# Attention, experts and FFN on one core: block sums one slot later, the first weights' load and its parts moved, ScalarE's order in step 1 changed

## The reference

```python
k_sum = k.reshape(B, H, nb, 32, D).max(axis=3)      # nb = 24 blocks of 32 keys
v_sum = v.reshape(B, H, nb, 32, D).mean(axis=3)
# scores: 1/8 q k^T where |i-j| < 16, else -1e9; and 1/8 q k_sum^T + log(32)
# softmax over both, times [v, v_sum]            -> x (1536 tokens, 512)
out = sum_e p[:, e] * (relu(x @ w1[e]) @ w2[e])     # 4 experts, hidden 1024
h = out @ w_in ; g = h * sigmoid(1.702 h) ; result = g @ w_out   # hidden 2048
```

## Time and profile before

| | |
|---|---|
| median of three runs | 845.85 us |
| the profiled execution's own time | 845.02 us |
| its span | 843.2 us |
| TensorE busy | 818.9 us |
| attention of the first sequence (slots) | 0 to 50.5 us |
| steps 0 and 1 on TensorE | 50.5 to 86.9 us |
| steps 2 to 47 and the end | 86.9 to 843.2 us |

### The profile page before, as it was taken

The page is one execution under the profiler, slowest core; times in us unless marked ns, Lnnn a source line. Parts: engine busy times, 40 slices in busy tenths (PEclk is TensorE's granted clock), DMA queues, the critical chain, the costliest instruction groups (busy, mean ns, idle before and its releaser), DMA issues.

```text
span 843.2 us, 13851 instructions
## 1 busy us (share of the span) xinstructions
PE 818.9 (97%) x5014; PEld 805.1 (95%) x5014; DVE 542.0 (64%) x1194; ACT 399.1 (47%) x859; POOL 555.5 (66%) x414
## 2 busy tenths in 40 slices
PE   5896999999999999999999999999999999999998
PEld 4786999999999999999999999999999999999998
DVE  6896666656665566566566666666676665665665
ACT  3863544544444454434334344444455555454541
POOL 3685566656566699756656578877578887466450
PEclk9978999999999999999999999999999999999999
DMA  9981216142112112212213112112112112322102
GB/s 265 277 218 57 92 54 216 51 149 73 51 63 108 51 51 93 77 51 98 72 51 108 62 51 101 51 50 101 51 51 101 50 55 96 126 68 84 51 1 76
DMA packets 26420, 74.72 MB, mean 89 GB/s; under 512 B 14704, under 2 KB 15856, under 8 KB 20208
## 3 DMA queue, kind: packets, MB, share of 16 engines
q1 hardware_dynamic: 26352, 73.84, 26.9%
HBM read 70.66 MB, written 3.17 MB: 88 GB/s over the span
## 4 chain that ended last, share of the span: by engine, by line
PE 89%; POOL 3%; SPq 3%; issue 1%; DMA 1%; DVE 1%; ACT 1%; DVEq 0%; ACTq 0%; POOLq 0%
PE bank L1146 29%; PE bank L1148 29%; PE bank L1147 29%; DMA v_cols<-v_t 1%; PE bank L1101 1%; SPq L404 1%; PE bank L1138 1%; PE bank L1112 1%; SPq L411 1%; POOL wd_lo L543 0%; POOL wd_lo L559 0%; POOL xb_other_lo L567 0%; POOL w_sum L520 0%; SPq L422 0%; SPq L417 0%
## 5 line engine op out<-in xcount | busy, mean ns | idle before, releaser
L948 DVE TENSOR_TENSOR xa<-bank,xa 128x384 f32<-128x384 f32 x352 | 195.8, 557 | 220.0 <-PE bank L1148 215.6
L1146 PE MATMUL bank<-h_hi,wd_hi 128*128 128x384 f32 x768 | 257.8, 336 | 0.1
L1148 PE MATMUL bank<-h_lo,wd_hi 128*128 128x384 f32 x768 | 257.4, 335 | 0.0
L1147 PE MATMUL bank<-h_hi,wd_lo 128*128 128x384 f32 x768 | 257.3, 335 | 0.0
L543 POOL TENSOR_TENSOR wd_lo<-stage,wd_hi 128x1024 fp32r<-128x1024 f32 x47 | 112.5, 2393 | 169.1 <-ACT wd_hi L714 169.1
L755 ACT ACTIVATE h_hi<-bank 128x384 fp32r<-128x384 f32 x192 | 94.3, 491 | 226.0 <-DVE bank L981 178.7
L1146 PEld LDWEIGHTS bank<-h_hi,wd_hi 128*128 128x128 f32 x768 | 144.7, 188 | 1.2 <-issue 1.2
L1147 PEld LDWEIGHTS bank<-h_hi,wd_lo 128*128 128x128 f32 x768 | 144.7, 188 | 0.0
L1148 PEld LDWEIGHTS bank<-h_lo,wd_hi 128*128 128x128 f32 x768 | 144.7, 188 | 0.0
L531 POOL TENSOR_TENSOR wu_lo<-stage,wu_hi 128x1024 fp32r<-128x1024 f32 x47 | 112.6, 2396 | 0.0
L1146 PE MATMUL bank<-xb_other_hi,wu_hi 128*128 128x384 f32 x336 | 112.3, 334 | 0.3 <-ACT snap L739 0.3
(11 more groups left out here) (79 smaller groups left out, 1283.2 us busy)
## 6 DMA issues: line engine op xcount, KB each, us to landing
stage<-weights SPq DMA_DIRECT2D x48, 1024.0 KB, 4.9
k_win<-k_w SPq DMA_DIRECT2D x8, 720.0 KB, 8.9
v_win<-v_w SPq DMA_DIRECT2D x8, 576.0 KB, 9.1
q_bd<-q_t SPq DMA_DIRECT2D x16, 192.0 KB, 8.8
p_bc<-p_rows SPq DMA_DIRECT2D x8, 384.0 KB, 4.8
v_cols<-v_t SPq DMA_DIRECT2D x6, 384.0 KB, 6.0
out<-xa SPq DMA_DIRECT2D x4, 384.0 KB, 7.5
out<-xa SPq DMA_DIRECT2D x8, 192.0 KB, 1.9
```

Of the source, the lines that this page charges most:

```text
L948: nc.vector.tensor_tensor(at, y_bank(g, t), at, ALU.add).then_inc(y_taken, 1)
L1146: nc.tensor.matmul(dst, w_h, a_h, start=first, stop=False, skip_group_check=True)
L1147: nc.tensor.matmul(dst, w_l, a_h, start=False, stop=False, skip_group_check=True)
L1148: return nc.tensor.matmul(dst, w_h, a_l, start=False, stop=last, skip_group_check=True)
```

## The change

Four edits; the instructions stay the same, their order changes.

1. **Block sums of values.** A new list `values_due(slot, lag)` sets the slots: the sum of unit u > 0 goes from slot 3u+1 to 3u+2, the turn and the mean from 3u+2 to 3u+3; the spread stays in 3u+4. Unit 0 is unchanged.
2. **Weights of pair 0.** Their load is issued behind `v_cols` and `v_win` of unit 3 and no longer ahead of them. `high_raw(0)` goes from slot 10 to slot 12, `low_first(0)` and `(1)` from slots 11, 12 to 13, 14, `high_down(0, *)` from slot 13 to 14, and `low_first(2)`, `(3)` from slots 14, 15 into step 0, behind `low_sums(1)`.
3. **ScalarE in step 1.** `keep(1, 1)` goes ahead of the exponentials of group 12, `high_raw(2)` from ahead of them to behind `high_hidden(1, "C11")` and `high_moved(0, 5)`.
4. **VectorE in step 1.** `low_moved(4)` goes up to the end of step 0, ahead of `add_c11(1)`; `value_sums(4)` goes up ahead of `take_y(0, 1)`, and `low_hidden(1, "C11")` behind it.

```diff
+        def values_due(slot, lag):
+            return [u for u in range(KT) if slot - lag == GROUPS * u + L_SUM + (u > 0)]
...
@@ SyncE
-            load_weights(0)
             load_value_columns(3)
             load_value_windows(3)
+            load_weights(0)
             sp.wait_ge(dp_done, 1)
...
@@ GpSimd
-                if slot in (11, 12):
-                    low_first(slot - 11)
-                if slot in (14, 15):
-                    low_first(slot - 12)
+                if slot in (13, 14):
+                    low_first(slot - 13)
...
+                if g == 0:
+                    low_first(2)
+                    low_first(3)
                 if g + 1 < STEPS:
                     low_down(g + 1)
@@ ScalarE
-                if slot == 10:
+                if slot == 12:
                     high_raw(0)
-                if slot == 12:
                     high_moved(0, 0)
                 if slot == 13:
                     high_moved(0, B12)
+                if slot == 14:
                     high_down(0, 0)
                     high_down(0, 1)
...
                 if g == 1:
                     high_moved(0, 4)
                     high_down(1, 0)
                     high_down(1, 1)
+                    keep(1, 1)
                     exponent(B_GROUPS)
+                    high_hidden(1, "C11")
+                    high_moved(0, 5)
+                    high_raw(2)
+                else:
...
@@ VectorE
             sum_first(4)
+            low_moved(4)
...
                     take_y(0, 0)
-                    low_moved(4)
+                    value_sums(KT)
+                    take_y(0, 1)
                     low_hidden(1, "C11")
-                    take_y(0, 1)
                     invert_sums(B_GROUPS)
                     take_y(0, 2)
                     low_moved(5)
                     take_y(0, 3)
-                    value_sums(KT)
```

More of the change, by code:

```diff
@@ L597, in _ @@
                     spread_key_maxima(u)
[L598 to L601, removed]
+                for u in values_due(slot, 2):
                     if u:
                         spread_value_means(u, norm_done, slot - L_NORM + 1)
-                if slot in (11, 12):
-                    low_first(slot - 11)
-                if slot in (14, 15):
-                    low_first(slot - 12)
+                    else:
+                        spread_value_means(u, kwin_done, 2)
+                if slot in (13, 14):
+                    low_first(slot - 13)
             for g in range(STEPS):
@@ L764, in _ @@
                         copy_prob_t(k)
-                for u in unit_starting(slot, L_MEAN):
+                for u in values_due(slot, 1):
                     value_means(u)
-                if slot == 10:
+                if slot == 12:
                     high_raw(0)
-                if slot == 12:
                     high_moved(0, 0)
@@ L795, in _ @@
                     high_down(1, 1)
+                    keep(1, 1)
                     exponent(B_GROUPS)
[L797 to L803, removed]
-                        exponent(k)
[L805 to L809, removed]
+                    high_hidden(1, "C11")
+                    high_moved(0, 5)
+                    high_raw(2)
+                else:
+                    if more:
+                        high_raw(g + 1)
+                    if ffn:
+                        sigmoid(g, "C11")
+                    high_hidden(g, "C11")
+                    for k in step_group(g):
+                        exponent(k)
+                    for k in step_group(g - 1):
+                        take_x(k)
+                    keep(g, 1)
                 if more:
@@ L1008, in _ @@
                     key_maxima(u)
-                for u in unit_starting(slot, L_SUM):
+                for u in values_due(slot, 0):
                     value_sums(u)
```

## The result

The changed kernel takes 838.22 us (median of 4 runs, 837.94 to 838.32) where the kernel before took 845.61 (4 runs, 844.2 to 846.78): a ratio of 0.9913, 95% interval 0.9896 to 0.993, so 7.4 us faster. The forecast was 842.3 us with a range from 838.4 up: the direction was right, the size half of what was measured. The profiled execution took 838.27 us, with a span of 836.5.

The account below looks back on a forecast made before the run. TensorE was taken as the bound, working 818.9 of 843.2 us. Reordering at -4.0 plus clock 0.5 gave -3.5 us: 841.5 from the profiled 845.02, plus 0.8 for the median, 842.3 us; range 838.4 to 846.2.

Parts of the forecast that it names:

- The bound and its size: TensorE bounds the kernel; step 1 holds 5.3 + 2.9 + 1.5 = 9.7 us: P7's stall, half clock, the turn's wait.
- Slots: In the slots the 1.79 us wait for `v_cols` goes; first tile at 49.5 instead of 50.52, gain 1.0 us.
- The walk: The prediction's operation-by-operation schedule through slots and steps 0 and 1, with step 2 at 82.8 instead of 86.86 us.
- Step 0: In step 0, GpSimd ends `low_first(3)` at 63.6; down(0,0), due at 62.4, waits 1.2 us, spending the first gain.
- the step that failed: In step 1, `low_down(1)` takes the turn before `sum_first(4)`; P7 begins at 68.65 instead of 72.19, 3.5 us earlier.
- rival B: In step 1, `sum_first(4)` precedes `low_down(1)` and `low_moved(5)` precedes `low_raw(2)`: about -6.5, 839.3 us; chance 0.14.
- the term of 0.5 us: In step 1, a clock still at half speed beyond 77.1 us costs 0.5 us, at most 5.6.
- The second load: Pair 2's weights, issued at 63.7, land at 70.2; `keep(1, 2)` ends at 74.3, hidden by 4 us.
- Two starts: In step 1, `low_down(1)` and `sum_first(4)` start within 0.15 us of one another.
- A: The case as worked out, clock low for a part of step 1: -2.6 to -5, 842.3 us; chance 0.50.

Follow-up runs that it names:

- the kernel with `high_down(1)` first: The changed kernel with high_down(1, 0) and (1, 1) ahead of high_moved(0, 4) on ScalarE, the run that forces the other order; 840.22 us, ratio 0.9935.
- `normalize(12)` first: The changed kernel with normalize of group 12 ahead of low_raw(2) on GpSimd instead of behind it; 836.91 us, ratio 0.9897.

## Why the prediction was half right

**The bound and its size: right.** The text put 9.7 us of possible gain into step 1 (stall, half clock, turn) and said that an offset won there lasts. 6.4 us of it came (36.34 to 29.97 between first tile and step 2), and all of it lasted. Edits 3 and 4 alone give it.

**Slots: the mechanism right, the gain of 1.0 us not there.** The wait for `v_cols` went, and pair 0's weights were hidden as said. The forecast had VectorE 1 us behind in slot 9; it was 1.4, or 1.8 counted from the masks of group 2 below, by the masks of group 7 in the kernel before and in the changed one:

```profile
30.05 0.27 DVE L880 CUSTOM_DVE_ANT_0 masked<-bank,cst 128x120 f32<-128x120 f32 x1
```

```profile
31.44 0.27 DVE L888 CUSTOM_DVE_ANT_0 masked<-bank,cst 128x120 f32<-128x120 f32 x1
```

First tile 50.13 for a forecast 49.5: 0.4 us instead of 1.0. Even these 0.4 us are luck: the masks of group 2, ahead of everything that was moved, began at 14.47 for 14.90 before, and from there to the first tile it is 35.7 us for 35.6. So edits 1 and 2 together won nothing in the slots, as the run with them alone says too (ratio 0.9997). The walk named the delay by edit 1 and had it won back by slot 12; by the pair of traces above it stays.

**Step 0: wrong.** A wait of 1.2 us was put on down(0,0), for `low_first(3)` at 63.6. It ended at 62.58 and down(0,0) was due at 63.06. GpSimd's own work was right, but of the 15.2 us with the turns it took 13.6 (from 49.03): one of the six turns of VectorE, `sum_first(3)` of 0.87 us, fell behind `low_first(3)` instead of ahead of it, and the other five cost 0.7 us each.

**Step 1: the step that failed.** "GpSimd, however, has been waiting since 64.35 with `low_down(1)` ... and takes the turn": in fact `sum_first(3)` ended at 63.4, so ScalarE's `high_moved(0, 4)` and `high_down(1, *)` ran a full us later than in the walk, `low_down(1)` was free only at 65.39, and `sum_first(4)` had begun at 64.19. It was rival B, given 0.14, that came. The trace of the kernel before had this order, by 1.2 us, and with the same releaser, `high_down(1, *)`:

```profile
64.42 0.95 DVE L932 TENSOR_TENSOR xa<-xa 128x768 f32<-128x768 f32 x1
...
65.63 2.37 POOL L543 TENSOR_TENSOR wd_lo<-stage,wd_hi 128x1024 fp32r<-128x1024 f32 x1 [4.61 <-ACT wd_hi L714]
```

By the run that forces the other order this is worth 1.8 us of the 2.7 us by which step 2 came before the forecast 82.8. The rest is `low_moved(5)`, which at 71.18 got its turn ahead of `low_raw(2)` (71.34) where the walk had it behind. It let down(0,5) begin at 72.72 instead of 77.1, but 1.38 us of that went into the wait of the transposes for `normalize`, which the walk doesn't have.

**The clock: the term of 0.5 us was zero.** In step 1 waits of 0.6, 0.2 and 1.4 us left it at full, and waits of 1.6, 0.9 and 1.3 us in the kernel with `high_down(1)` first; with edit 3 alone, waits of 1.9 and 1.8 us brought it down. By the Trainium skill's rule on idle gaps (TensorE: Matmul & The Clock Gate, section "HAM oscillation — how this bites in real kernels") none of these should. The fall with edit 3 doesn't agree with that, so the doubt about the rule was right and the price put on it here was not. What the walk left out is the clock at the other end: in the changed kernel it came back 1.0 us into the first tile for 0.2 before, which loses 0.4 us.

**The second load: hidden, as said.** It was issued at 62.60 (forecast 63.7), 11 us later than before, and landed 4.9 us later (forecast 6.5), at 67.5, ahead of GpSimd's need at 68.2. So GpSimd began pair 2's sums 2.0 us earlier than the walk's 70.2.

**The range.** It began at 838.4, 0.2 us above the median measured. Two starts lay 0.15 us apart in the walk, and the walk's own error at that point was already 0.6 us; so A and B deserved like chances, and the range had to include all of B.

## What to carry to other kernels

This walk through a schedule was off by half a us to one us after 30 us; where it decides between two orders that lie closer than that, both orders are cases of equal weight and their difference is the width of the range. Where VectorE and GpSimd take turns, the release time of the operation that would wait is what to trace back (here ScalarE's order), not its length, and the rows of the kernel before, where they hold the same pair, are the first thing to compare with. A reordering in several places is worth splitting on the chip: of four edits here two carried all, the other two together gave nothing, one of them costs about 1 us by the traces, and a fifth that the change doesn't have, `normalize(12)` first, is worth another 1.6 us between first tile and step 2.

## What the runs showed of the hardware that was not expected

- The clock fell at 73.2 us in the kernel with edit 3 alone though no wait of TensorE in step 0 or 1 before it was longer than 1.94 us.
- How long the clock stays at half after the slots varies from kernel to kernel, from 0.2 to 4.0 us into the first tile, which is worth up to 1.9 us and stands in no wait.
- A down product that is released 0.1 us after it is due shows no idle time in the rows and still loses 0.3 us. down(0,3) of the changed kernel was due at 69.42, and `take_y(0, 1)` ended at 69.53. It starts 0.33 us after the matmul ahead of it, and its second matmul 0.28 us later, where 0.17 is the pitch:

```profile
69.25 0.34 PE L1156 MATMUL bank<-h_lo,wd_hi 128*128 128x384 f32 x1
69.58 0.44 PE L1154 MATMUL bank<-h_hi,wd_hi 128*128 128x384 f32 x1
69.86 0.34 PE L1155 MATMUL bank<-h_hi,wd_lo 128*128 128x384 f32 x1
```

- Loads in the slots vary as much as the largest gain here: the first tile of two kernels with the same slots began at 49.15 and at 55.55 us.
- An operation of VectorE that reads a single small tile takes turns with GpSimd too, so the prediction's "two operands in SBUF" is too narrow. In the kernel before it takes 0.17 us here and 1.43 us at 44.74, beside GpSimd's copy:

```profile
30.86 0.17 DVE L890 TENSOR_SCALAR row_sum_e<-row_sum 128x4 f32<-128x4 f32 x1
```
